# Six expert blocks of batches 0 and 1 computed inside the attention tiles of batches 2 and 3

## The chip, the core and the metric

One core of a Trainium2 chip runs the whole kernel. Its engines are TensorE (PE; its weight loads are listed as PEld), VectorE (DVE), ScalarE (ACT), GpSimd (POOL) and SyncE (SP, which here only issues DMAs). Each takes its instructions in order and waits on semaphores. The metric is the device time of one execution in microseconds (us); lower is better.

## The reference, cut to what matters

Three stages follow each other: attention, an expert layer, and a mixer. The first two:

```python
# attention: 4 batches, 8 heads, 576 tokens, head size 64
scores = scale * q @ k.T
kth = 32nd largest of each row          # only scores >= kth stay
x = softmax(scores where >= kth) @ v
# experts: per token, in order of the sequence of each batch
logits = x @ w_gate                     # 8 experts
fresh_e = argmax(logits[s])
e = fresh_e if s == 0 or sigmoid(x @ w_local) < 0.5 else prev_e
p = softmax(logits[s])
y[s] = p[e] * (relu(x[s] @ w1[e]) @ w2[e])   # 512 -> 1024 -> 512
```

The expert of a token depends on that of the token before it in its batch, and never on another batch. The mixer (a Fourier transform over tokens and channels, a normalisation and a two-layer network) reads y and is the same in both kernels.

## The kernel before, in words

**Attention** (`attention`). Batches 0 and 1 are worked on together, head by head, then batches 2 and 3. That makes 16 units (`NPAIR`) of 9 tiles of 128 query rows each, 144 tiles (`NTILE`). In each unit tiles 0 to 3 belong to the first batch, 5 to 8 to the second, and the middle one, 4, holds 64 rows of each; it comes last. For tile t: PE computes 576 scores per row (L179), ACT copies them to SBUF (L289), DVE finds the 32 largest by seven operations, four MAX8 (L356) and three MATCH_REPLACE8 (L358), POOL builds the mask (L332) and applies it (L336) to the exponentials that ACT made (L282), PE turns the result over (L199, L201), ACT copies that out (L271, L273), and PE multiplies with the values (L227). DVE works on two tiles in alternation, `top_op(c, n)` with c the pair of tiles and n from 0 to 13. After each turn PE runs four matmuls of the identity whose result nobody reads (`keep_clock`, L210). The order on each engine is the loop `body(t)` in `run`: at step t, PE does the turn of tile t, then for even t+5 the scores of the tiles t+5 and t+6 (`LQ` = 5), then the values of tile t-1. Six buffers hold scores (`NS`). Once in nine tiles PE also computes the gates (L242).

**Routing** (`routing`). When attention has ended, DVE and PE turn the logits into a table: for each block of 128 slots of one expert, which tokens it gathers and with which gate. `NBLK` is 25, the most blocks there can be.

**Experts** (`experts`). Block by block, POOL gathers 128 rows of x from DRAM, PE turns them over (L771) and computes the hidden layer (L783), ACT and DVE split hidden values and weights into two parts each, PE computes the output in three products (L796 to L798), and POOL scatters it to `y_d` and, in reverse row order, to `r_d`. The first `SURE` = 18 blocks always run; each later one runs if the routing made so many blocks.

**Weights.** SP loads those of experts 0 and 7 (8 MB, L664 and L670) at the start, and in `experts` those of the next expert when a block's expert differs from that two blocks earlier.

Of the kernel before, what the change touches and what calls it, by code (L numbers as in the profile page):

```python
# [34 lines left out]
PAD = 1 << 20  # L35
C_IM8, C_SEG, C_J, C_LATER, C_TILE = 0, E, E + E * NT, E + E * NT + NBLK, E + E * NT + NBLK + NT
C_PAD, C_ROW, C_EPS, C_POS, C_ONE, C_UP, C_ODD, CST = 240, 270, 288, 290, 418, 546, 674, 700


def attention(nc, env, q_h, k_h, v_h, vt_h):  # L40
# [4 lines left out]
    LQ, LE = 5, 2  # L45
    NS, NE, NT_ = 6, 3, 3
    ORDER = [r for p in range(MID) for r in (p, p + MID + 1)] + [MID]
# [3 lines left out]
    with ExitStack() as ctx:  # L51
# [23 lines left out]
        ps_s = [pb(f"ps_s{n}", [P, 2, 512]) for n in range(2)]  # L75
# [12 lines left out]
        s_norm = [sem(f"s_norm{b}") for b in range(2)]  # L88
        block = ctx.enter_context(nc.Block(no_gpsimd_drain=True))
        LAST = NTILE - TPP  # L90

        @block.sync
        def _(sp):
# [42 lines left out]
            for c in range(2):  # L136
                load_w1(sp, env, (0, E - 1)[c], c)
                load_w2(sp, env, (0, E - 1)[c], c)
            with sp.Fori(1, NPAIR // 2) as i:
                for b in range(2):  # L140
                    sp.wait_ge(s_qk, TPP * (2 * i + b - 1))
                    load_qk(2 * i + b, b)
                    load_mid(2 * i + b, b)
                    sp.wait_ge(s_vw, 2 * i + b - 1)
                    load_vt(2 * i + b, b)
                    sp.wait_ge(s_pv, TPP * (2 * i + b - 1))
                    load_v(2 * i + b, b)
            for m in range(NT):
                bb, r = m // TPP, m % TPP if m < TPP else ORDER[m % TPP]
                n = bb * TPP + r  # L150
                sp.wait_ge(s_norm[bb], m % TPP + 1)
                sp.dma_start(env["x_d"][n * P:(n + 1) * P, :], X[:, r, bb * DM:(bb + 1) * DM]).then_inc(env["s_xd"], 16)

        def normalise(eng, r, bb):
            x = X[:, r, bb * DM:(bb + 1) * DM].rearrange("p (h d) -> p h d", h=H)
            eng.tensor_tensor(x, x, den[:, r, H * bb:H * bb + H, None].broadcast_to([P, H, D]), ALU.mult).then_inc(s_norm[bb], 1)

        def run(body):
            for t in range(-LQ, NTILE + 2):
                body(t)  # L160
# [8 lines left out]
        def _(pe):  # L169
            def score(k, h):  # L170
                b, r = (k // TPP) % 2, ORDER[k % TPP]
                if r < MID:
                    lhsT, rows = q_sb[b][0:D, r * P:(r + 1) * P], slice(0, D)
                elif r > MID:
                    c0 = (P - HALF) + (r - MID - 1) * P
# [3 lines left out]
                return pe.matmul(ps_s[k % 2][:, h, 0:SH], lhsT, k_sb[b][rows, h * SH:(h + 1) * SH], start=True, stop=True)  # L179

            def scores(k):
                for n in (k, k + 1):
                    b, p = (n // TPP) % 2, n % TPP
                    if p == 0:
                        pe.wait_ge(s_qk_in[b], 32 * (n // (2 * TPP) + 1))
                    if ORDER[p] == MID:
                        pe.wait_ge(s_mid_in[b], 32 * (n // (2 * TPP) + 1))
                if k >= 2:
                    pe.wait_ge(s_copy, k)
                score(k, 0)  # L190
                score(k + 1, 0)
                score(k, 1).then_inc(s_qk, 1)
                score(k + 1, 1).then_inc(s_qk, 1)
# [18 lines left out]
            def values(k):  # L212
                b, r = (k // TPP) % 2, ORDER[k % TPP]
                if r == 0:
# [9 lines left out]
                lo, hi = (0, VW) if r < MID else (VW, 2 * VW) if r > MID else (0, 2 * VW)  # L224
# [20 lines left out]

            def body(t):
                if live(t):
# [14 lines left out]
        def _(act):  # L262
            act.dma_start(k_sb[0][:, :], k_h[0]).then_inc(s_qk_in[0], 16)

            def body(t):
# [19 lines left out]
                if live(k):  # L285
                    act.wait_ge(s_qk, (k | 1) + 1)
                    if k >= NS:
                        act.wait_ge(s_mask, k - NS + 1)
                    act.activation(s_sb[k % NS][:, :].rearrange("p (h c) -> p h c", h=2), ps_s[k % 2][:, :, 0:SH],  # L289
                                   ACT.Copy).then_inc(s_copy, 1)  # L290
                k = t - 1
                if live(k):
                    u, r = k // TPP, ORDER[k % TPP]
                    act.wait_ge(s_pv, k + 1)
                    for two in range(2):
                        if (two == 0 and r > MID) or (two == 1 and r < MID):
                            continue
                        rows = slice(0, P) if r != MID else slice(two * HALF, two * HALF + HALF)
                        c0 = two * VW
                        act.activation(gd[rows, r, u, :], ps_o[k % 2][rows, c0 + D:c0 + VW], ACT.Copy)  # L300
                        op = act.activation(X[rows, r, u * D:(u + 1) * D], ps_o[k % 2][rows, c0:c0 + D], ACT.Copy)  # L301
                    op.then_inc(s_o, 1)
                if gates_at(t):
# [5 lines left out]
                    act.activation(g[0:S - KC * P, KC], src[0:S - KC * P, KC], ACT.Copy).then_inc(s_vg, 1)  # L309

# [1298 lines left out]
```

## Time and profile before

| | us |
|---|---|
| median of 3 runs | 1561.29 |
| lowest and highest | 1560.42, 1561.83 |
| profiled execution | 1560.65 |
| its span, first to last instruction | 1558.8 |
| PE busy | 1417.2 (91%) |
| DVE busy | 1075.7 (69%) |
| ACT busy | 604.3 (39%) |
| POOL busy | 624.9 (40%) |
| mean granted clock of PE | 0.926 |

Busy time is an average over stages with different limits. In time, the attention's last search for maxima ends at 703.4 us, routing's first operation is at 720.0, the first block's transposes are at 743.1, the mixer's first loads are issued at 1041.0, and the span ends at 1558.8. The stage at hand has to be read by itself, from the timeline and from windows. The clock is listed as a share of 2.4 GHz: 1.00 is 2.4 GHz throughout, 0.50 is 1.2 GHz throughout.

### The profile page before, as it was taken

How to read it: one execution, taken by the hardware profiler on the slowest of the kernel's cores; microseconds unless marked ns; L12 is line 12 of the kernel's file. 1: busy time of each engine (PE TensorE's matmuls, PEld its weight loads, DVE VectorE, ACT ScalarE, POOL GpSimd, SP SyncE). 2: the span in 40 equal slices, each digit the busy share in tenths (PEclk: the TensorE clock that was granted, in tenths of full speed). 3: DMA queues.
4: the chain of work that ended last, by engine and by line, in shares of the span. 5: the costliest groups of instructions: out<-in, count | busy, mean ns of one | idle time of the engine just before them, and what ended most of it. 6: DMA issues, size and time to landing. Idle time of an engine off the chain costs nothing. (4 is left out here: it accounts for less than half of the span.)

```text
span 1558.8 us, 24264 instructions
## 1 busy us (share of the span) xinstructions
PE 1417.2 (91%) x8476; PEld 1214.2 (78%) x8476; DVE 1075.7 (69%) x2133; ACT 604.3 (39%) x1469; POOL 624.9 (40%) x502
## 2 busy tenths in 40 slices
PE   6898898989888998985999999967999999999998
PEld 4777777777677777774899999953777789999987
DVE  7999999999999999998455555546646422422222
ACT  4555455555455555541444444413322221321111
POOL 4666666666866666660244444422202100000000
PEclk9889898898999988986899999975999999999999
DMA  9110111111011011102017356442322011411111
GB/s 324 34 33 28 29 32 32 33 32 28 14 31 32 25 32 32 69 1 75 32 59 260 132 193 234 160 153 89 128 75 71 31 41 65 138 41 41 41 41 61
DMA packets 67146, 117.01 MB, mean 75 GB/s; under 512 B 27283, under 2 KB 27412, under 8 KB 67042
## 3 DMA queue, kind: packets, MB, share of 16 engines
q1 hardware_dynamic: 57306, 87.19, 16.9%
q0 software_dynamic: 8928, 27.00, 4.9%
q8 instruction: 60, 0.98, 0.3%
q10 hardware_dynamic: 808, 1.48, 0.3%
q14 instruction: 44, 0.36, 0.1%
HBM read 87.33 MB, written 30.42 MB: 76 GB/s over the span
## 5 line engine op out<-in xcount | busy, mean ns | idle before, releaser
L332 POOL TENSOR_SCALAR keep<-s_sb,top 128x576 f32<-128x576 f32 x142 | 244.4, 1721 | 224.2 <-DVE top L356 224.2
L356 DVE MAX8 top<-w_sb 128x8 f32<-128x576 f32 x432 | 304.0, 744 | 0.0
L227 PEld LDWEIGHTS ps_o<-v_sb,eT 128*128 128x128 f32 (+1 forms) x1440 | 202.0, 206 | 37.7 <-issue 26.3
L227 PE MATMUL ps_o<-v_sb,eT 128*128 128x74 f32 (+3 forms) x1440 | 225.4, 298 | 0.0
L1367 DVE SCALAR_TENSOR_TENSOR h_lo<-ps_ch,h_hi 128x384 fp32r<-128x384 f32 x96 | 53.4, 556 | 242.1 <-ACT h_hi L1218 242.0
L358 DVE MATCH_REPLACE8 w_sb<-top,w_sb 128x576 f32<-128x576 f32 x288 | 211.2, 739 | 0.0
L336 POOL TENSOR_TENSOR e_sb<-e_sb,keep 128x576 f32<-128x576 f32 x142 | 200.0, 1408 | 21.8 <-POOL keep L332 0.6
L199 PE MATMUL ps_t<-ident,e_sb 128*128 128x128 f32 x576 | 107.0, 315 | 84.4 <-POOL e_sb L336 78.7
L210 PE MATMUL ps_o<-ident 128*128 128x128 f32 x1152 | 180.5, 309 | 0.0
L210 PEld LDWEIGHTS ps_o<-ident 128*128 128x128 f32 x1152 | 167.1, 223 | 1.9 <-ACT rows L301 0.7
L783 PEld LDWEIGHTS ps_h<-bxT,w 128*128 128x128 f32 x1408 | 162.4, 194 | 3.4 <-issue 1.6
L783 PE MATMUL ps_h<-bxT,w 128*128 128x128 f32 x1408 | 162.7, 277 | 1.2 <-SPq L755 1.2
L1218 ACT ACTIVATE h_hi<-ps_ch 128x384 fp32r<-128x384 f32 x96 | 47.1, 491 | 286.6 <-PE ps_ch L1050 286.6
L199 PEld LDWEIGHTS ps_t<-ident,e_sb 128*128 128x128 f32 x576 | 68.3, 155 | 102.7 <-POOL e_sb L336 91.5
L271 ACT ACTIVATE eT<-ps_t 128x512 f32<-128x512 f32 x144 | 86.0, 597 | 140.2 <-PE ps_t L199 140.1
L1048 PE MATMUL ps_ch<-un_hi,w_hi 128*128 128x384 f32 x384 | 132.0, 344 | 1.6 <-DVE un_lo L1361 1.6
L1050 PE MATMUL ps_ch<-un_hi,w_lo 128*128 128x384 f32 x384 | 130.1, 339 | 0.0
L1049 PE MATMUL ps_ch<-un_lo,w_hi 128*128 128x384 f32 x384 | 129.6, 338 | 0.0
L824 ACT ACTIVATE w_hi<-w 128x1024 fp32r<-128x1024 f32 x88 | 85.8, 1045 | 102.8 <-PE ps_y L798 101.8
L289 ACT ACTIVATE s_sb<-ps_s 128x576 f32<-128x576 f32 x144 | 92.1, 640 | 81.5 <-PE ps_s L179 81.5
L282 ACT ACTIVATE e_sb<-s_sb,nmax 128x576 f32<-128x576 f32 x144 | 111.9, 777 | 14.3 <-ACT nmax L277 1.5
L1048 PE MATMUL ps_cy<-w_hi,h_hi 128*128 128x512 f32 x288 | 114.3, 397 | 0.0
(214 smaller groups left out, 2409.9 us busy)
## 6 DMA issues: line engine op xcount, KB each, us to landing
w<-in_w SPq DMA_DIRECT2D x18, 2048.0 KB, 13.5
stage<-in_w_ch SPq DMA_DIRECT2D x16, 512.0 KB, 3.5
q_sb<-in_q SPq DMA_DIRECT2D x16, 288.0 KB, 2.8
vT<-in_vt SPq DMA_DIRECT2D x16, 288.0 KB, 3.1
x_d<-rows SPq DMA_DIRECT2D x18, 256.0 KB, 2.4
u<-u_d SPq DMA_DIRECT2D x18, 256.0 KB, 2.9
x_d<-u POOLq DMA_DIRECT2D x18, 256.0 KB, 2.6
u<-x_d SPq DMA_DIRECT2D x18, 256.0 KB, 2.8
```

What stands on the lines that cost most here:

```text
L199: mm = pe.transpose(ps_t[:, c * P:(c + 1) * P], e_sb[k % NE][:, c * P:(c + 1) * P], ident[:, :])
L210: pe.matmul(ps_o[k % 2][:, 384:384 + P], ident[:, :], ident[:, :], start=True, stop=True)
L227: mm = pe.matmul(ps_o[k % 2][:, lo:hi], eT[k % NT_][0:n, c, :], v_sb[b][0:n, c, lo:hi], start=(c == 0), stop=(c == KC))
L282: act.activation(e_sb[k % NE][:, :], s_sb[k % NS][:, :], ACT.Exp, bias=nmax[:, k % NE:k % NE + 1], scale=SCALE).then_inc(s_exp, 1)
L332: pool.tensor_scalar(keep[t % 2][:, :], s_sb[t % NS][:, :], top[t % NS][:, TOPK - 1:TOPK], None, ALU.is_ge).then_inc(s_keep, 1)
L336: pool.tensor_tensor(e_sb[t % NE][:, :], e_sb[t % NE][:, :], keep[t % 2][:, :], ALU.mult).then_inc(s_mask, 1)
L356: dve.max(eight, src).then_inc(s_top, 1)
L358: dve.match_replace(out=w_sb[k % 2][:, :], in_to_replace=eight, in_values=src, imm_value=-BIG).then_inc(s_top, 1)
L783: mm = pe.matmul(ps_h[half][:, m, :], w1[c][:, k, f0:f0 + P], xT[c][:, k, :], start=(k == 0), stop=(k == NC - 1))
L1048: pe.matmul(out_, hi1, hi2, start=first, stop=False)
L1049: pe.matmul(out_, hi1, lo2, start=False, stop=False)
L1050: return pe.matmul(out_, lo1, hi2, start=False, stop=last)
```

## The change

Four things are new in `attention`. The routing of batches 0 and 1 (tokens 0 to 1151) is computed by a generator, `early_routing`, of which DVE takes two steps after each `top_op` from pair 38 on. PE's part of it stands at fixed places of the tiles 74 to 79 (`HOPS`). From tile 83 to 142 PE runs 105 small units, spread evenly: for each of 6 blocks (`NA`) the turn of x ("x"), 8 units of the hidden layer ("h", four matmuls of 128x128 each) and 8 of the output ("y", one matmul of 128x512), in plain float32; `keep_clock` stops at tile 83. The blocks are laid out full ones first, then partly filled ones. ACT copies the units' results and issues the loads of their weights, with the expert read from SBUF; POOL gathers and scatters.

The two banks of PSUM that the units need come from the scores: each tile has one bank now instead of two, half of a pair's scores is computed at each step, and ACT copies them in two pieces of 288 instead of one of 576. Batches 0 and 1 are normalised in the tiles 75 to 79, two a tile, and stored at once. The routing after attention treats the tokens of the second half, and gives slots of the full table to those of the first half that are in none of the six blocks. `SURE` is 12 now. The weights of experts 0 and 7 for the expert stage are loaded by ACT near the end of attention instead of by SP at the start.

```diff
+    HOPS = [(MIDDLE + n, at) for n, at in ((2, 2), (3, 2), (4, 1), (4, 2), (5, 2), (7, 2))]
...
-        ps_s = [pb(f"ps_s{n}", [P, 2, 512]) for n in range(2)]
+        ps_s = [pb(f"ps_s{n}", [P, 512]) for n in range(2)]
+        ps_a = [pb(f"ps_a{n}", [P, 512]) for n in range(2)]
...
+        UNITS = [("x", 0, 0)] + [("none", 0, 0)] * 3
+        for j in range(NA):
+            UNITS += [("h", j, m) for m in range(NF)] + [("y", j, m) for m in range(NF // 2)]
+            UNITS += [("x", j + 1, 0)] if j + 1 < NA else []
+            UNITS += [("y", j, m) for m in range(NF // 2, NF)]
+        EARLY0, EARLY1 = MIDDLE + 11, NTILE - 1
...
             def body(t):
                 if live(t):
                     if t == 0:
                         pe.wait_ge(env["s_ident"], 1)
                     turn(t)
-                    keep_clock(t)
-                if live(t + LQ) and (t + LQ) % 2 == 0:
-                    scores(t + LQ)
+                    if t < EARLY0:
+                        keep_clock(t)
+                between(t, 0)
+                k = t + LQ
+                if live(k):
+                    scores(k - k % 2, k % 2)
+                between(t, 1)
                 if live(t - 1):
                     values(t - 1)
+                between(t, 2)
...
+                if t == MIDDLE + 7:
+                    act.wait_ge(a["s_idx"], IDX_E)
+                    for j in range(2):
+                        early_w1(j)
+                        early_w2(j)
+                for unit in units_at(t):
+                    early(*unit)
...
+                if t == EARLY0 - 1:
+                    pool.wait_ge(a["s_idx"], IDX_G)
+                    pool.wait_ge(env["s_xd"], 16 * HT)
+                    for j in range(2):
+                        gather(j)
...
+            routing = early_routing()
             for c in range(NTILE // 2):
                 for n in range(14):
                     top_op(c, n)
-                if c == NTILE // 4 + 2:
-                    dve.wait_ge(s_o, NTILE // 2)
-                    invert(slice(0, TPP), 0)
+                    now[0] = (c, n)
+                    if c >= ROUTE:
+                        next(routing, None)
+                        next(routing, None)
...
-        SURE = NT
+        SURE = NT - NA
```

(`units_at(t)` gives the units of tile t, the n-th of them at place n modulo 3; `MIDDLE` is 72, `ROUTE` 38.)

The order on PE at tiles 89 and 90, before: `ps_t` is the turned tile, `ps_o` identity products and values, `ps_s` scores.

```order
L199 MATMUL ps_t<-ident,e_sb 128x128 x4
L201 MATMUL ps_t<-ident,e_sb 64x128
L210 MATMUL ps_o<-ident 128x128 x4
L179 MATMUL ps_s<-k_sb,q_sb 128x288 x4
L227 MATMUL ps_o<-v_sb,eT 128x74 x5
L199 MATMUL ps_t<-ident,e_sb 128x128 x4
L201 MATMUL ps_t<-ident,e_sb 64x128
L210 MATMUL ps_o<-ident 128x128 x4
L227 MATMUL ps_o<-v_sb,eT 128x148 x5
```

The same place now; `ps_a` takes the units' results, `stage` and `w_0` are their inputs:

```order
L363 MATMUL ps_t<-ident,e_sb 128x128 x4
L365 MATMUL ps_t<-ident,e_sb 64x128
L448 MATMUL ps_a<-stage,w_0 128x128 x4
L345 MATMUL ps_s<-k_sb,q_sb 128x288 x2
L448 MATMUL ps_a<-stage,w_0 128x128 x4
L391 MATMUL ps_o<-v_sb,eT 128x74 x5
L363 MATMUL ps_t<-ident,e_sb 128x128 x4
L365 MATMUL ps_t<-ident,e_sb 64x128
L458 MATMUL ps_a<-w_0,stage 128x512
L345 MATMUL ps_s<-k_sb,q_sb 128x288 x2
L458 MATMUL ps_a<-w_0,stage 128x512
```

The identity products are gone, four unit pieces stand in their place, and the scores are two and two instead of four at once.

The order on DVE at the start of a pair of tiles in the second half, before:

```order
L356 MAX top<-w_sb 128x8 x2
L358 MATCH_REPLACE w_sb<-top,w_sb 128x576 x2
L356 MAX top<-w_sb 128x8 x2
L358 MATCH_REPLACE w_sb<-top,w_sb 128x576 x2
L356 MAX top<-w_sb 128x8 x2
```

And now, at the start of pair 40, where the generator counts the slots of each expert:

```order
L682 MAX top<-s_sb 128x8
L733 CAST early_cnt<-ps_a 128x8
L734 TENSOR_SCALAR early_cnt<-ps_a 128x8
L682 MAX top<-s_sb 128x8
L735 TENSOR_SCALAR early_cnt<-early_cnt 128x16
L736 TENSOR_TENSOR early_cnt<-early_cnt 128x8
L684 MATCH_REPLACE w_sb<-top,s_sb 128x576
L738 SCALAR_TENSOR_TENSOR early_endb<-cst,early_cnt 128x16
L740 TENSOR_SCALAR early_full<-early_cnt 128x8
L684 MATCH_REPLACE w_sb<-top,s_sb 128x576
L741 TENSOR_TENSOR early_move<-early_endb 128x8
L742 SCALAR_TENSOR_TENSOR early_move<-early_move,early_full 128x8
```

Between one search operation and the next, two steps of the routing stand.

The order on ACT at the end of tile 79, before (`gd` and `rows` are the copies of a tile's result, `v_sb` the gates' columns):

```order
L300 ACTIVATE gd<-ps_o 128x10
L301 ACTIVATE rows<-ps_o 128x64
L308 ACTIVATE v_sb<-ps_o 128x8x9
L309 ACTIVATE v_sb<-ps_o 64x2x9
L271 ACTIVATE eT<-ps_t 128x512
L273 ACTIVATE eT<-ps_t 64x128
```

And now, where ACT reads the first blocks' experts and loads their weights:

```order
L549 ACTIVATE rows<-ps_o 128x64
L556 ACTIVATE v_sb<-ps_o 128x8x9
L557 ACTIVATE v_sb<-ps_o 64x2x9
L572 TENSOR_LOAD early_e
L572 ISA x2
L1040 ISA
L1040 DMA w_0<-in_w 128x4x1024
L580 TENSOR_LOAD early_e
L580 ISA x2
L1046 ISA
L1046 DMA w_0<-in_w 128x8x512
L572 TENSOR_LOAD early_e
```

Four such groups (two blocks, two weights each) stand between tile 79's copies and the next tile's.

## Rows read from the trace of the kernel before

**Rows 1.** Page, span in 40 slices: busy tenths, and granted clock in tenths.
```profile
PE   6898898989888998985999999967999999999998
...
PEclk9889898898999988986899999975999999999999
```

**Rows 2.** Groups by line: line, engine, op, tiles, count | busy us, mean ns | idle, releaser.
```profile
L356 DVE MAX8 top<-s_sb 128x8 f32<-128x576 f32 x144 | 100.8, 740 | 8.3 <-ACT s_sb L289 8.3
...
L783 PE MATMUL ps_h<-bxT,w 128*128 128x128 f32 x1408 | 162.7, 277 | 1.2 <-SPq L755 1.2
```

**Rows 3.** Windows of one pair of tiles: busy by engine, PEclk, DMA share.
```profile
481.10:490.80 9.70, 7.18 (x56) 6.14 (x56) 9.70 (x21) 5.04 (x15) 6.24 (x4) 1.00 0.00 0
...
548.60:558.20 9.60, 7.49 (x38) 6.92 (x38) 9.60 (x21) 3.32 (x10) 6.23 (x4) 0.64 0.01 2
...
sum 298.80, PE 263.48 PEld 223.40 DVE 298.80 ACT 156.64 POOL 199.35; mean PE 8.50 PEld 7.21 DVE 9.64 ACT 5.05 POOL 6.43
```

**Rows 4.** Timeline, two tiles at the full clock: start, length, engine, line, op, tiles.
```profile
567.55 0.66 PE L199 MATMUL ps_t<-ident,e_sb 128*128 128x128 f32 x4
...
568.15 1.06 PE L210 MATMUL ps_o<-ident 128*128 128x128 f32 x8
...
568.42 1.39 DVE L356 MAX8 top<-s_sb 128x8 f32<-128x576 f32 x2
...
569.14 1.24 PE L179 MATMUL ps_s<-k_sb,q_sb 64*128 64x288 f32 x8
...
570.31 1.49 PE L227 MATMUL ps_o<-v_sb,eT 128*128 128x74 f32 x10
...
571.72 0.66 PE L199 MATMUL ps_t<-ident,e_sb 128*128 128x128 f32 x4
...
573.22 1.38 PE L227 MATMUL ps_o<-v_sb,eT 128*128 128x74 f32 x10
...
574.53 0.66 PE L199 MATMUL ps_t<-ident,e_sb 128*128 128x128 f32 x4
...
578.06 1.39 DVE L356 MAX8 top<-s_sb 128x8 f32<-128x576 f32 x2
```

**Rows 5.** Timeline of PE: gates; scores of a pair with the middle tile.
```profile
578.71 1.29 PE L242 MATMUL ps_o<-wg_sb,vT 128*128 128x18 f32 x10
...
682.15 0.75 PE L179 MATMUL ps_s<-k_sb,q_sb 64*128 64x288 f32 x2
...
684.78 1.38 PE L227 MATMUL ps_o<-v_sb,eT 128*128 128x74 f32 x10
```

**Rows 6.** Timeline of PE in the experts: the next block's transposes, twice.
```profile
1002.23 0.60 PE L771 MATMUL ps_bx<-ident,x 128*128 128x128 f32 x4
...
1015.27 0.60 PE L771 MATMUL ps_bx<-ident,x 128*128 128x128 f32 x4
```

**Rows 7.** Timeline of DVE: logits, and small operations of routing.
```profile
705.49 0.83 DVE L369 TENSOR_TENSOR part<-gd,den 128x648 f32<-128x648 f32 x1
...
706.35 1.31 DVE L371 TENSOR_REDUCE lg<-part 128x81 f32<-128x648 f32 x1
...
726.74 0.17 DVE L604 TENSOR_SCALAR cnt_i<-cnt_i 128x8 int32<-128x8 int32 x1
...
726.95 0.18 DVE L605 TENSOR_TENSOR_SCAN endb<-cst,cnt_i 128x8 f32<-128x8 f32 x1
...
727.44 0.30 DVE L608 SCALAR_TENSOR_TENSOR place<-endb,ps_r 128x144 f32<-128x144 f32 x1
```

**Rows 8.** Timeline of SP's queue: weight loads issued back to back.
```profile
14.73 0.51 SPq L670 DMA_DIRECT2D w<-in_w  x1
...
15.28 5.65 SPq L664 DMA_DIRECT2D w<-in_w  x1
...
20.98 2.44 SPq L670 DMA_DIRECT2D w<-in_w  x1
```

**Rows 9.** Timeline of PE, last tiles of attention.
```profile
696.58 1.12 PE L199 MATMUL ps_t<-ident,e_sb 128*128 128x128 f32 x4 [3.50 <-POOL e_sb L336]
```

More of the change, by code:

```diff
@@ L88, in attention, with units_at, unit_tile @@
         s_norm = [sem(f"s_norm{b}") for b in range(2)]
+        s_rt = sem("s_rt")
+        r, a = choice_buffers(nc, ctx, "_a", ps_a), early_buffers(nc, ctx, env)
+        a["s_yo"] = env["s_early"]
         block = ctx.enter_context(nc.Block(no_gpsimd_drain=True))
         LAST = NTILE - TPP
+        cst = env["cst"]
+        ones, below = cst[:, C_ONE:C_ONE + P], cst[:, C_UP:C_UP + P]
+        NF = F // P
+        UNITS = [("x", 0, 0)] + [("none", 0, 0)] * 3
[4 more added lines that the diff above has]
+        EARLY0, EARLY1 = MIDDLE + 11, NTILE - 1
+        def units_at(t):
+            at = lambda x: min(max(len(UNITS) * (x - EARLY0) // (EARLY1 - EARLY0), 0), len(UNITS))
+            return UNITS[at(t):at(t + 1)]
+        def unit_tile(unit):
+            return next(t for t in range(EARLY0, EARLY1) if unit in units_at(t))
         @block.sync
@@ new lines, in early_inverse, with early_x @@
+            def early_inverse():
+                pe.wait_ge(r["s_go"], WHAT)
+                for n in range(HT):
+                    pe.wait_ge(r["s_go"], POS + n + 1)
+                    mm = pe.matmul(ps_a[1][:, 0:2 * NA], a["at_pos"][:, n, :], a["what"][:, n, :, :].rearrange("p a j -> p (a j)"),
+                                   start=(n == 0), stop=(n == HT - 1))
+                mm.then_inc(r["s_back"], 1)
+            def early_x(j, bank):
+                pe.wait_ge(a["s_x"][j % 2], 16 * (j // 2) + 16)
+                if j > 0:
+                    pe.wait_ge(a["s_h"], 2 * j)
+                else:
+                    pe.wait_ge(a["s_idx"], IDX_GATE)
+                for k in range(KC):
+                    mm = pe.transpose(bank[:, k * P:(k + 1) * P], env["x"][j % 2][:, k * P:(k + 1) * P], ident[:, :])
+                mm.then_inc(a["s_t"], 1)
@@ new lines, in between @@
+            def between(t, at):
+                if (t, at) == HOPS[0]:
+                    choice_turn(pe, r, ident)
+                elif (t, at) == HOPS[1]:
+                    choice_ends(pe, r, ident)
+                elif (t, at) == HOPS[2]:
+                    choice_row(pe, r, ones)
+                elif (t, at) == HOPS[3]:
+                    choice_last(pe, r, ident)
+                elif (t, at) == HOPS[4]:
+                    early_rank()
+                elif (t, at) == HOPS[5]:
+                    early_inverse()
+                for n, unit in enumerate(units_at(t)):
+                    if n % 3 == at:
+                        early(*unit)
@@ L404, in _ @@
                     op.then_inc(env["s_lg"], 1)
-            for r in ORDER[early:]:
-                normalise(dve, r, 1)
+            for rt in ORDER[early:]:
+                normalise(dve, rt, 1)
 def wait_apart(eng, s, value, idle):
```

559 lines of the change are left out of this document (408 added, 151 removed).

## The prediction

> **What bounds the kernel now.** I read the slices first. In the attention, the first 18 of 40 slices, PE's digits are 8 and 9 and its clock's too [rows 1], so both PE and DVE look full. The groups by line settle which of them sets the pace. The searches for maxima never wait except once, 8.3 us at the start [rows 2]; windows of 9.6 us show DVE busy for all of each and PE for 8.50 of 9.64 on the mean [rows 3]. One pair of tiles takes DVE 578.06 - 568.42 = 9.64 us [rows 4], and 72 pairs make 694 us. DVE bounds the attention, and work that is put on it there costs its full length.
>
> In the experts it is PE: two blocks' transposes stand 1015.27 - 1002.23 = 13.04 us apart [rows 6], with no gap of PE between. The hidden layer's group has 1408 instructions [rows 2] at 64 a block (two for each float32 matmul, 32 matmuls), so 22 blocks run. The mixer comes after all of this and is not touched.
>
> **Blocks that go.** The tables are decided by the inputs. By the reference on the drawn inputs the tokens of the eight experts are 418, 244, 288, 356, 217, 167, 276, 338, which makes 22 blocks, as the trace has. Of batches 0 and 1 they are 242, 119, 157, 178, 78, 77, 147, 154. The six blocks are the full ones of experts 0, 2, 3, 6 and 7 and the partly filled one of expert 0, with 114. What is left is 176, 244, 160, 228, 217, 167, 148, 210: two blocks each, 16. Six blocks go, 6 x 13.04 = -78.2 us. More expert changes stall only if loads come late; the loads come every fourth block, while a load of two weights has the time of about a block and a half, as before. The nine conditional blocks that are skipped at the end, three before, cost some branches beside a POOL that is still scattering: 0 to 1 us, I take 0.3.
>
> **DVE in the attention.** The generator adds 69 operations (the inversion of the sums was in the loop before). Two are the logits, from after the loop: 0.86 us from the one's start to the other's [rows 7], and 1.31. The other 67 are small. In routing such an operation takes 0.17 to 0.18, and 0.21 from start to start in a dependent row [rows 7]; those with 128x144 outputs take 0.30, and here they are 128x72. I count 30 narrow ones at 0.18, 28 at 0.24 (half-width tables, reductions, scans) and the 9 comparisons with 128 positions at 0.22: 14.1 us. With the logits +16.3. From below, an operation lies partly under the next: two searches of 0.74 [rows 2] take 1.39 together [rows 4], so 0.05 to 0.09 of each could hide: 12. From above, each waits for the one before it, +0.06 each: 21. PE's answers that DVE waits for are due one to several searches later than PE can reach its place by my count from pair 37 on, so I charge nothing for them; 3 if one is late. The logits' old place at the end lay beside PE's last tiles and gives nothing back.
>
> **PE in the attention, tiles 83 to 142.** This is the term on which all hangs. At the full clock, a pair takes PE 574.53 - 567.55 = 6.98 us, of which the identity products are 569.14 - 568.15 = 0.99 a tile [rows 4]. That leaves 5.00. Gates add 1.29 in nine tiles [rows 5], 0.29 a pair. A middle tile among the scores makes them 684.78 - 682.15 = 2.63 [rows 5] instead of 570.31 - 569.14 = 1.17 [rows 4], 0.32 a pair. A "h" unit is 8 instructions of the hidden layer, 8 x 162.7/1408 = 0.92 us [rows 2]; a "y" unit has as many columns and fewer weight loads, so 0.92 at most; turning x is 0.6 [rows 6]. A block is 16 x 0.92 + 0.6 = 15.3 us, six are 92, over 30 pairs 3.06. Two groups of scores a pair instead of one cost one more change of row groups, 0.2. Sum: 5.00 + 0.29 + 0.32 + 3.06 + 0.2 = 8.9 us, against 9.64 of DVE. It fits by 0.7 us a pair, at the full clock.
>
> How much delay does DVE bear? The second half of a pair's scores is computed now at the even tile, after POOL's mask of that tile. From the timeline I place the copy about 6 us after the start of the pair before, so about 3.5 us ahead of need. A lag of PE under 3.5 us is free, and what is longer stalls DVE.
>
> The clock decides whether it fits. Before, single pairs show 1.00, and one shows 0.64 [rows 3]; the page's digits are 8 and 9 [rows 1]. The drop near the end comes after PE waited 3.50 us for POOL [rows 9]. With PE busy for more of each pair, waits of that kind get shorter. I take the clock at about 0.97, at which 8.9 becomes 9.2, and charge 5 us for pairs in which gates, middle tile and a low stretch meet. From below 0. From above, a pair at 0.82 would take 10.9, 1.2 us over DVE's, 36 us over 30 pairs.
> The Trainium skill ("TensorE: Matmul & The Clock Gate", on what actually happens) has the clock fall after idling and return with sustained work. The row of the 3.50 us wait agrees, and by that rule this term would be 0.
>
> **ACT and the weight loads.** ACT issues four loads of 2 MB in a row at tile 79. On SP's queue such issues took 0.51 us, then 5.65 and 2.44 [rows 8]: an issue can hold its engine. ACT executes in order, so eT of tile 80, the exponential of tile 82 and the scores of pair 42 queue behind it; PE waits for the first, POOL for the second, DVE for the third. ACT is free for them between 2 and 11 us after the expert numbers come, which are due early in pair 41; pair 42 starts some 11 us later. I take a stall of 3, of 0 to 6. Later loads come one at a time and take 0.5.
> The Trainium skill ("DMA: Bandwidth & Descriptors", on issuing engines that are no separate queues) calls the time to initiate a DMA usually small beside the DMA. The row of 5.65 us speaks against it; by the rule this term would be 0.
>
> The scores' copy is two of 288 columns instead of one of 576, one more instruction a tile on an engine that is busy for 5.05 of 9.64 us [rows 3]: nothing. POOL has 9.64 - 6.43 = 3.2 idle us a pair [rows 3], which holds two normalisations or a gather.
>
> **Ends.** At the start PE's second half waits for ACT's copies of the first: +0.7 (0 to 1.5), a copy and a short matmul group. At the end, tiles 140 to 142 carry six "y" units, 5.5 us, where four tiles had 4 x 0.99; the clock is low there after the wait of 3.50 us [rows 9], which doubles part of it, and ACT issues the last load before it copies tile 143: +3 (0 to 6). Routing afterwards works on half-width tables but with the same number of steps: 0 (-2 to +1).
>
> **The sum.** -78.2 + 0.3 + 16.3 + 5 + 3 + 0.7 + 3 = -49.9. The profiled execution took 1560.65, so 1510.8; the median before is 1561.29, 0.6 higher. I forecast 1511.
>
> **Rivals.**
> (a) PE becomes the bound in the tiles 83 to 142. For it: only 0.7 us of 9.64 is spare, and the mean over windows before is 8.50 busy with less work [rows 3]. Against it: those 8.50 include low clock and identity products. If the clock stays at about 0.86 there, a pair takes 10.3, +20 us: about 1531. Chance 0.17.
> (b) Slower than before. The same mechanism with the low clock for most of the stretch: without the identity products, PE waits at each even mask, falls to half speed, and works at it for the rest of the pair. It decides against the change from the point where a pair costs 50/30 = 1.7 us more than forecast, 11.3 us, a mean clock of 0.79. At 0.72 a pair is 12.4 and the kernel 1589. For it: a pair at 0.64 exists [rows 3]. Against: in the next highest idle case, 7.18 busy, the clock was 1.00. Chance 0.03.
> (c) The stage of experts does not shrink as said: a block more is left (rounding in the logits moves a token over an edge), or ifs and weight loads stall PE. Of what is left, expert 1 with 244 is nearest to a third block, 13 tokens away. One block is +13: 1524. Chance 0.03.
> (d) It is cheaper than I say: the added operations hide better and PE never lags: -78.2 + 12 + 3 = 1497. Chance 0.15.
> The forecast itself, 1503 to 1520, has 0.62.
>
> **Numbers.** The range that holds 8 in 10 takes in most of the cheap case (d) and of (a), whose upper bound of 36 us would end at 1542: 1494 to 1540. A measurement of this kernel can tell 0.2%, 3 us, from no change. Only (b) ends above 1558, and a part of it between: faster 0.95, same 0.01, slower 0.04.
>
> **What would show it.** In the profile after: 16 blocks, 1024 instructions of the hidden layer, 13.0 us apart. The last search ends near 703 + 25 = 728. Small operations between the searches sum to 16 us in the pairs 38 to 42. In the second half of the tiles, windows show DVE busy for all or nearly all of each pair; if its searches wait for ACT's scores by more than 10 us in sum, (a) holds, and the granted clock of the stretch tells whether by clock or by work. A gap of ACT right behind the four loads shows their price. What would make it wrong most easily is PE's sum of 8.9: a few tenths more in each pair take all the spare time.

## The result and the profile after

| | before | after |
|---|---|---|
| median, us | 1560.86 (1559.59 to 1561.83) | 1522.06 (1512.85 to 1523.24) |
| ratio of the times | 1 | 0.9741, 95% interval 0.9707 to 0.9775 |
| profiled execution, its span | 1560.65, 1558.8 | 1512.85, 1511.0 |
| mean granted clock of PE, profiled | 0.926 | 0.933 |

The change takes 38.8 us off the median; the forecast was 1511, in a range of 1494 to 1540. So the time lies in the range, but the gain is 11 us short of the forecast's 49.9. The profiled execution, 1512.85, is the fastest of the four, and the other three took 1521.2 to 1523.2 at a mean clock of 0.923 to 0.926 (two more on record, not in the median, took 1517.3 and 1524.4). So there are two questions: what the trace is made of, and what it does not contain.

The page of the changed kernel, PE's busy tenths and its granted clock in 40 slices, answers [rows 1]:

```profile
PE   6889889989879999999679999847999999999998
...
PEclk9989998998779999999779999956999999999999
```

The two sevens in a row early on are the 11th and 12th slice, 378 to 453 us. There the early routing runs, between the searches of the tiles 76 to 83. From there to the end of the attention the clock is 9 or more.

The groups by line, the ones that answer to [rows 2] and the two new ones of the units:

```profile
L682 DVE MAX8 top<-s_sb 128x8 f32<-128x576 f32 x144 | 103.2, 769 | 10.7 <-ACT s_sb L538 10.6
...
L1159 PE MATMUL ps_h<-bxT,w 128*128 128x128 f32 x1024 | 119.5, 278 | 1.2 <-SPq L1131 1.2
...
L448 PE MATMUL ps_a<-stage,w 128*128 128x128 f32 x384 | 53.6, 283 | 0.0
L458 PE MATMUL ps_a<-w,stage 128*128 128x512 f32 x96 | 51.0, 618 | 0.0
```

The hidden layer has 1024 instructions, 16 blocks. The searches waited 10.6 us for score copies, 8.5 of them at the start; only 2.07 are new. A search reads 769 ns in place of 740, yet a pair of tiles takes what it took. Windows of one pair of tiles each in the second half answer to [rows 3]:

```profile
477.33:486.97 9.64, 9.64 (x61) 6.79 (x59) 9.64 (x22) 6.16 (x20) 6.24 (x5) 1.00 0.41 141
544.79:554.43 9.64, 8.30 (x52) 5.77 (x50) 9.64 (x22) 5.16 (x17) 6.25 (x5) 1.00 0.08 29
...
670.10:679.74 9.64, 9.64 (x50) 6.19 (x50) 9.64 (x22) 4.91 (x17) 6.25 (x5) 1.00 0.51 198
```

DVE is busy for the whole of each pair, the clock is 1.00, and a pair is 9.64 us as before. PE reads as full in two of them and is still not the bound: the searches never wait here, and a run below puts PE's own work at 8.9 us a pair.

Where the new waits are, in a list of DVE's waits from 370 to 750 us (what waits, for whom, us in total, times, longest):

```profile
DVE early_cnt L733 <- PE ps_a L415: 2.2, 1, 2.2
DVE spread_a L127 <- PE ps_a L81: 2.1, 1, 2.1
DVE top L682 <- ACT s_sb L538: 2.1, 1, 2.1
...
DVE early_oh L133 <- PE ps_a L87: 0.4, 1, 0.4
```

Three are the early routing's waits for PE, 4.75 us, and the fourth stands behind ACT's four weight loads. Their timeline:

```profile
427.04 0.24 ACT L556 ACTIVATE v_sb<-ps_o 128x72 f32<-128x72 f32 x1 [10.25 <-PE ps_o L406]
...
428.41 0.43 ACTq L1040 DMA_DIRECT2D w<-in_w  x1
429.56 0.40 ACTq L1046 DMA_DIRECT2D w<-in_w  x1
430.65 3.17 ACTq L1040 DMA_DIRECT2D w<-in_w  x1
434.51 2.09 ACTq L1046 DMA_DIRECT2D w<-in_w  x1
436.71 0.60 ACT L518 ACTIVATE eT<-ps_t 128x512 f32<-128x512 f32 x1 [9.38 <-issue]
```

The experts' blocks are 13.04 us apart, as in [rows 6]:

```profile
776.43 0.60 PE L1147 MATMUL ps_bx<-ident,x 128*128 128x128 f32 x4
...
789.47 0.60 PE L1147 MATMUL ps_bx<-ident,x 128*128 128x128 f32 x4
```

And the stage's end, the last scatter of POOL and the first loads of the mixer, first the changed kernel, then the kernel before:

```profile
981.19 0.97 POOL L1257 DMA_INDIRECT r_d<-y,at_y  x1 [0.30 <-issue]
992.36 1.99 SPq L1346 DMA_DIRECT2D xa<-y_d  x3
```

```profile
1037.58 0.98 POOL L881 DMA_INDIRECT r_d<-y,at_y  x1 [0.30 <-issue]
1041.00 1.30 SPq L970 DMA_DIRECT2D xa<-y_d  x3
```

From 982.16 to 992.36 are 10.2 us, where before there were 2.4. PE's last matmul had ended at 977.7, and no engine has a row in those 10.2 us. This is called the gap below.

The traces side by side, by milestones:

| stretch | before | after | difference | forecast |
|---|---|---|---|---|
| to the first search | 7.86 | 8.56 | +0.7 | +0.7 |
| first search to the last one's end | 695.6 | 719.5 | +23.9: 17.1 operations, 4.75 waits for PE, 2.07 behind ACT | +16.3, 0, +3, and +5 for PE |
| last search to routing's first operation | 16.5 | 13.7 | -2.8 | +3 |
| routing, to the first block | 23.1 | 22.7 | -0.4 | 0 |
| experts, to the end of POOL's last scatter | 295.5 | 217.7 | -77.8 | -78.2 |
| gap before the mixer | 2.4 | 10.2 | +7.8 | +0.3 |
| mixer | 517.8 | 518.7 | +0.8 | 0 |
| span | 1558.8 | 1511.0 | -47.8 | -49.9 |

### The profile page after: what moved, and what is told of

It reads as the page before. It is cut to its first block and busy times, and to the rows that moved or that the text cites. A ratio compares the mean times of both kernels' runs of the same rounds, so it can differ in the third digit from the quotient of the medians.

```text
span 1511.0 us, 23165 instructions
## 1 busy us (share of the span) xinstructions
PE 1376.4 (91%) x7974; PEld 1127.9 (75%) x7974; DVE 1049.7 (69%) x2158; ACT 596.6 (39%) x1596; POOL 613.8 (41%) x493
## 3 DMA queue, kind: packets, MB, share of 16 engines
q8 instruction: 65, 1.06, 0.3%
## 5 line engine op out<-in xcount | busy, mean ns | idle before, releaser
L682 DVE MAX8 top<-w_sb 128x8 f32<-128x576 f32 x432 | 311.3, 774 | 0.1
L391 PEld LDWEIGHTS ps_o<-v_sb,eT 128*128 128x128 f32 (+1 forms) x1440 | 191.7, 195 | 59.9 <-issue 47.2
L391 PE MATMUL ps_o<-v_sb,eT 128*128 128x74 f32 (+3 forms) x1440 | 217.4, 290 | 0.0
L363 PE MATMUL ps_t<-ident,e_sb 128*128 128x128 f32 x576 | 100.9, 301 | 63.9 <-POOL e_sb L659 52.3
L345 PE MATMUL ps_s<-k_sb,q_sb 64*128 64x288 f32 x512 | 119.5, 496 | 7.0 <-DMA k_sb<-in_k 4.6
L1159 PEld LDWEIGHTS ps_h<-bxT,w 128*128 128x128 f32 x1024 | 119.2, 195 | 2.9 <-issue 1.6
L1159 PE MATMUL ps_h<-bxT,w 128*128 128x128 f32 x1024 | 119.5, 278 | 1.2 <-SPq L1131 1.2
L538 ACT ACTIVATE s_sb<-ps_s 128x288 f32<-128x288 f32 x288 | 104.8, 406 | 38.8 <-PE ps_s L345 38.3
L1426 PE MATMUL ps_cy<-w_hi,h_lo 128*128 128x512 f32 x288 | 113.3, 394 | 0.0
L1425 PE MATMUL ps_cy<-w_lo,h_hi 128*128 128x512 f32 x288 | 113.1, 393 | 0.0
## 6 DMA issues: line engine op xcount, KB each, us to landing
w<-in_w SPq DMA_DIRECT2D x12, 2048.0 KB, 10.9
```

The costliest lines, as they stand in the source:

```text
L345: return pe.matmul(ps_s[k % 2][:, 0:SH], lhsT, k_sb[b][rows, h * SH:(h + 1) * SH], start=True, stop=True)
L363: mm = pe.transpose(ps_t[:, c * P:(c + 1) * P], e_sb[k % NE][:, c * P:(c + 1) * P], ident[:, :])
L391: mm = pe.matmul(ps_o[k % 2][:, lo:hi], eT[k % NT_][0:n, c, :], v_sb[b][0:n, c, lo:hi], start=(c == 0), stop=(c == KC))
L682: dve.max(eight, src).then_inc(s_top, 1)
L1159: mm = pe.matmul(ps_h[half][:, m, :], w1[c][:, k, f0:f0 + P], xT[c][:, k, :], start=(k == 0), stop=(k == NC - 1))
L1425: pe.matmul(out_, hi1, lo2, start=False, stop=False)
```

## Experiments

Each time is a median, and the kernel before, measured beside each, had medians of 1560.2 to 1560.5. The changed kernel itself came first.

**The changed kernel again.**

> The changed kernel once more, for a second trace. Its other executions stood 4 to 12 us above the profiled one (1512.85) with a lower mean granted clock (0.921 to 0.927 against 0.933). Theory A: in the slower ones the clock falls in more windows of tiles 83 to 142, PE's pair then passes 9.64 us and the searches wait: DVE's waits after 450 us rise from none to 5 to 10 us, and the last search ends at 733 to 738 instead of 728.0. Theory B: the attention is the same (728 within 1 us) and the difference lies in the mixer or the expert stage, the block distance staying 13.04. The gap from the end of POOL's last scatter (982.16) to the mixer's first loads (992.36) is 10.2 again by both.

Measured: 1519.71 (1509.53 to 1526.04), ratio 0.9754 (0.9730 to 0.9778). Its trace was again of the fastest execution, so it could decide nothing on the other runs. The gap was 9.3 us, not 10.2. Its waits for PE in the early routing were 1.2 us where the first trace had 4.75: that term moves from execution to execution.

**The skipped blocks.** Two kernels with nested conditional blocks, on all engines and on PE alone:

```diff
-            for j in range(SURE, NBLK):
-                with eng.If(used > j):
-                    body(j // 2, j % 2)
+            def rest(j):
+                with eng.If(used > j):
+                    body(j // 2, j % 2)
+                    if j + 1 < NBLK:
+                        rest(j + 1)
+
+            rest(SURE)
```

> Each conditional block from the 13th on stands inside the one before it, on all engines, so that one jump ends the stage where nine were taken. Theory A (the skipped blocks cost the 7.8 us that the gap before the mixer has grown by): the gap of 10.2 us falls to 2.4 or less, and the time falls by 7 to 8 us against the changed kernel in the same call. Theory B (the gap is the landing of the scatters or the stage's barrier): it stays at 10 us and the time is the same within 2 us.

> The same nesting on PE alone; DVE, ACT, POOL and SP still jump over nine blocks one by one. PE's last matmul ends at 977.7 and the mixer starts 14.7 us later, which is 1.6 us a skipped block if PE is the last; before it was 7.0 us for three, with POOL's scatter ending 2.4 us before the mixer. Theory A (PE's jumps set the end): the gap falls to 2.4 to 4 us, as with all engines nested. Theory B (POOL's own jumps behind its scatter set it, 0.9 us each): it stays at 10 us. If it falls by 1 to 5 us, two engines are near each other.

Measured: all engines 1504.08, ratio 0.9650 (0.9633 to 0.9667); PE alone 1507.16, 0.9679 (0.9649 to 0.9710). POOL's last scatter and the mixer's first loads, nested on all engines, then on PE alone:

```profile
979.78 0.97 POOL L1261 DMA_INDIRECT r_d<-y,at_y  x1 [0.30 <-issue]
983.30 1.42 SPq L1350 DMA_DIRECT2D xa<-y_d  x3
```

```profile
980.24 0.97 POOL L1266 DMA_INDIRECT r_d<-y,at_y  x1 [0.30 <-issue]
984.97 1.31 SPq L1355 DMA_DIRECT2D xa<-y_d  x3
```

The gap is 2.55 and 3.76 us. So PE's jumps made most of it, and those of the other engines are worth 1.2 us more. The control, nested on POOL alone:

> The nesting on POOL alone; PE jumps over nine blocks one by one, as in the changed kernel. Theory A (PE's jumps set the gap, and the repeated runs spread with them): the gap is 9 to 10.5 us, the median 1517 to 1521 and the highest run above 1522, as in the changed kernel and unlike the two kernels whose PE is nested (medians 1504.1 and 1507.2). Theory B (any change of the program's code removes the spread, or it was luck): the median is 1510 to 1513.

Measured: 1515.13 (1511.95 to 1517.59), ratio 0.9713 (0.9700 to 0.9727). The gap was 10.9 us (981.93 to 992.85): it stays, as theory A has it, 0.4 us over the range given. The median lies between the ranges of both theories, and no run was above 1518, so PE's jumps alone do not bring the spread of the repeated runs. The same question put to the kernel before:

```diff
+            for _ in range(more):
+                with eng.If(used > NBLK - 1):
+                    body((NBLK - 1) // 2, (NBLK - 1) % 2)
...
-            blocks(pe, used, body)
+            blocks(pe, used, body, more=6)
```

> The kernel before, with six more conditional blocks on PE alone, never taken, behind its own three. Theory A (PE jumps over a conditional block at 1.3 to 1.6 us each, and the kernel before hides three of them beside POOL's scatter): the gap from the end of POOL's last scatter to the mixer's first loads goes from 2.4 us to 10 us, and the time is 7 to 8 us above the kernel before. If the repeated runs spread by 10 us and more here as well, where those of the kernel before lie within 3.9 us (1558.67 to 1562.56), the spread too comes of the jumps. Theory B (the jumps were dear in the changed kernel only for its place in memory or its early blocks): the time is that of the kernel before within 2 us.

Measured: 1570.11 (1569.03 to 1570.65), ratio 1.0064 (1.0050 to 1.0078), which is 9.8 us more, and a spread of 1.6 us. In its trace:

```profile
1036.76 0.99 POOL L884 DMA_INDIRECT r_d<-y,at_y  x1 [0.30 <-issue]
1049.95 2.14 SPq L973 DMA_DIRECT2D xa<-y_d  x3
```

A gap of 12.2 us. PE's last matmul had ended at 1033.2; nine jumps and the stage's end took 16.8 us, and with three they took 7.0 at most (1034.0 to 1041.0, set by POOL's scatter). Six jumps are thus worth at least (16.8 - 7.0) / 6 = 1.6 us each. The jumps do not take the same time in every execution. With nine of them the time from PE's last matmul to the mixer's first loads is 12.8 to 16.5 us in the traces of the changed kernel and its variants (14.7 in the first one), and 7.0 with one, again set by POOL. In the first trace that makes between (14.7 - 7.0) / 8 = 1.0 and 14.7 / 9 = 1.6 us for each.

**The waits for PE in the early routing.** First by the clock, then by the order.

```diff
-                for _ in range(4):
+                for _ in range(12 if MIDDLE + 1 <= k < EARLY0 else 4):
```

> Twelve clock-keeping matmuls in place of four in each of tiles 73 to 82, nothing else. In the changed kernel DVE waited 2.12, 0.40 and 2.23 us for PE there (399.11, 402.61, 408.77) and PE itself 3.71 us for DVE, at a granted clock of 0.55 to 0.68. Theory A (the waits come of the low clock, that came of PE's idling while the searches of a pair take 13 to 16 us): the clock stays at 1.0 from 380 to 440 us, the waits fall from 4.75 us to under 1.5, and the last search ends 3 to 4 us earlier (724 to 725). Theory B (the waits are of the order of the instructions: each hop stands behind a turn and a values step): the waits stay at 4 to 5 us or rise by the 1 to 2 us that the added matmuls take.

Measured: 1521.83 (1516.64 to 1527.84), ratio 0.9764 (0.9729 to 0.9799). The waits did not fall: those for PE were 5.1 us (3.6 and 1.5), and those behind ACT rose to 5.8 over that stretch. But the clock was not held either. The windows of 380 to 390 and 410 to 420 us showed 1.00, 390 to 400 still 0.69, so this run does not part the two theories cleanly. The last search ended at 734.9; 2.7 us of that come from one pair of the first half, which took 12.35 us while PE was at 0.50 (it comes up again below). Then the places of the waits:

```diff
-    HOPS = [(MIDDLE + n, at) for n, at in ((2, 2), (3, 2), (4, 1), (4, 2), (5, 2), (7, 2))]
-    AWAIT = [(ROUTE + n, at) for n, at in ((0, 9), (1, 0), (1, 7), (1, 10), (2, 0), (3, 4))]
+    HOPS = [(MIDDLE + n, at) for n, at in ((2, 2), (3, 2), (4, 1), (4, 2), (5, 2), (8, 1))]
+    AWAIT = [(ROUTE + n, at) for n, at in ((0, 9), (1, 0), (1, 10), (1, 13), (2, 3), (3, 9))]
```

> The four later waits of DVE for PE's answers in the early routing stand three to five searches later, and PE's inversion two places later (tile 80 in place of 79); the rest is the changed kernel, whose two traces show 4.75 and 1.2 us of such waits (spread_a, early_oh, early_cnt) and its last search ending at 728.06 and 726.93. Theory A (the waits are of the order: the answer comes one to three searches after it is asked for, more when the clock is low; more clock-keeping matmuls made it worse): the three waits fall to under 0.5 us in sum, the last search ends at 725 to 726.5 with the wait behind ACT's loads (1.9 to 2.1 us) left, and the repeated runs, 1509.5 to 1526.0 for the changed kernel, lie closer, with a median 5 us or more lower. Theory B (the waits are not what makes the runs differ): the sum falls all the same but the median stays within 2 us of the changed kernel's 1519.7 to 1522.

Measured: 1518.18 (1514.81 to 1524.22), ratio 0.9741 (0.9720 to 0.9763). The three waits are gone, and one has grown, in DVE's waits of this kernel from 370 to 750 us:

```profile
DVE top L682 <- ACT s_sb L538: 5.0, 1, 5.0
```

The gain was given back: the five pairs from the 38th on took 73.32 us, and 73.33 in the changed kernel. The searches come to this place 2.8 us earlier, but the expert numbers that ACT waits for in tile 79 do not (426.9 us, 427.3 in the changed kernel), and ACT is through with its loads at 436.8 (436.7). That takes 2.9 us back; the other 1.8 went into operations that took longer. The last search ended at 729.0, not at the 725 to 726.5 of theory A, and by the median theory B holds. So both were taken together, with the nesting:

```diff
-                if t == MIDDLE + 7:
-                    act.wait_ge(a["s_idx"], IDX_E)
-                    for j in range(2):
-                        early_w1(j)
-                        early_w2(j)
+                if t == MIDDLE + 8:
+                    act.wait_ge(a["s_idx"], IDX_E)
+                    early_w1(0)
+                if t == MIDDLE + 9:
+                    early_w2(0)
+                if t == MIDDLE + 10:
+                    early_w1(1)
+                if t == MIDDLE + 11:
+                    early_w2(1)
```

> Together: the nested conditional blocks on all engines (1503.34 to 1508.72 by themselves), the later waits of the run hops, and ACT's four weight loads at tiles 80, 81, 82 and 83, one each, in place of all at tile 79. Theory A (each takes away its own wait): the wait of the searches for ACT's score copy (1.9 to 2.3 us in four traces) goes, the last search ends at 723.5 to 724.5, the gap before the mixer is 2.5 us, and the time is 1499 to 1501, 3 us below the nested kernel. Theory B (a load that comes later makes PE wait for the first expert's weights or for the gathered rows at tiles 83 to 85, and DVE with it): DVE has a new wait of 2 us or more between 430 and 460 us, and the time is that of the nested kernel, 1503 to 1506.

> The combined kernel again, for a trace without the long low-clock stretch: its first trace (1511.34) had PE at a clock of 0.50 from 254 to 288 us, a tile of PE at 6.78 us where the searches of a tile take 4.82, and three pairs of 12.49, 13.56 and 12.12 us; its other runs were 1499.24 to 1506.87. Theory A (that stretch alone set that run apart): a trace without it has all pairs up to 370 us at 9.64 us, the last search ends at 725 to 727, and the time is 1499 to 1502; a second trace with it lies 8 to 10 us above. Theory B: runs differ in the expert stage or the mixer, and a fast run has its last search at 735 as well.

Measured: 1502.38 (1499.24 to 1511.34), ratio 0.9619 (0.9603 to 0.9636), and 1501.08 (1499.57 to 1509.00), ratio 0.9635 (0.9615 to 0.9654). It is the fastest version here. The second trace is of 1499.57: DVE has no wait between 370 and 720 us, the five pairs take 69.18 us, the last search ends at 723.8, a little earlier than forecast, and the gap is 2.5 us.

The first trace is of the run at 1511.34, the only one of the longer runs that was seen from inside. Its last search ended at 735.2. Windows of half a pair from 249.64 us, and the five turns of PE in that stretch:

```profile
249.64:254.46 4.82, 3.11 (x19) 2.85 (x18) 4.82 (x11) 1.48 (x6) 4.52 (x4) 0.72 0.00 0
254.46:259.28 4.82, 4.82 (x18) 3.55 (x16) 4.82 (x11) 1.66 (x4) 1.71 (x2) 0.50 0.01 3
...
268.92:273.74 4.82, 4.82 (x20) 3.65 (x19) 2.05 (x5) 1.60 (x5) 4.38 (x3) 0.50 0.01 3
...
283.38:288.20 4.82, 4.82 (x20) 3.61 (x19) 2.83 (x7) 1.09 (x5) 3.10 (x2) 0.50 0.00 0
...
293.02:297.84 4.82, 4.82 (x38) 3.93 (x35) 2.45 (x6) 3.31 (x10) 3.26 (x3) 1.00 0.01 3
```

```profile
252.53 1.11 PE L363 MATMUL ps_t<-ident,e_sb 128*128 128x128 f32 x4 [1.71 <-POOL e_sb L663]
...
260.26 1.12 PE L363 MATMUL ps_t<-ident,e_sb 128*128 128x128 f32 x4
...
267.04 1.12 PE L363 MATMUL ps_t<-ident,e_sb 128*128 128x128 f32 x4
...
273.82 1.12 PE L363 MATMUL ps_t<-ident,e_sb 128*128 128x128 f32 x4
...
280.60 1.12 PE L363 MATMUL ps_t<-ident,e_sb 128*128 128x128 f32 x4
```

After a wait of 1.71 us for POOL, PE works at 0.50 (1.2 GHz) for 34 us of whole windows without a pause, about 41 us with the parts of the windows at both ends. A tile takes it 6.78 us, a pair 13.56, and the pairs of the searches take 12.49, 13.56 and 12.12 us there, 9.25 over three of 9.64. In the trace of the kernel nested on all engines the clock fell in the same place (0.50 from 254.46) and was at 0.94 from 264.10 on; no search waited. The shorter form is in the run with more clock-keeping: 0.50 in the windows from 138.32 to 152.78 us and 0.78 in the next, and its pair of 12.35 us.

**PE's spare time, and the clock-keeping.**

```diff
-                    if t < EARLY0:
-                        keep_clock(t)
+                    keep_clock(t)
```

> The changed kernel with the four clock-keeping matmuls a tile kept in tiles 83 to 143 too, beside the expert units. PE is busy 8.6 to 8.9 us of a pair's 9.64 there, and eight matmuls of a pair take 2.1 us at full clock (1.06 a tile). Theory A (PE has a spare of 0.7 to 1.0 us a pair and no more): a pair becomes 10.7 to 11.0 us, the 30 pairs take 32 to 41 us more, the last search ends at 760 to 768 us, and the time is 1545 to 1560. Theory B (part of PE's busy time is the lengthened reading of matmuls that stand in a queue, and the spare is larger): the last search ends below 745 us.

Measured: 1551.56 (1550.41 to 1555.43), ratio 0.9949 (0.9933 to 0.9965). The pairs from the 46th to the 69th took 261.41 us, 10.89 each at a clock of 1.00, and the last search ended at 759.3, 0.7 us short of the range. PE is busy in all windows of that stretch and the searches wait 31 us for score copies, so PE sets the pace there. Less the identity products, 0.99 in each of its two tiles, PE's pair is 8.9 us, the forecast's number. The opposite, no identity products in the first half of the combined kernel:

```diff
-                for _ in range(4):
+                for _ in range(4 if k >= MIDDLE else 0):
```

> The combined kernel without clock-keeping matmuls in tiles 0 to 71. At the low clock a tile of PE is 6.78 us, 1.92 of them clock-keeping, so without them 4.86 to 4.94, near the 4.82 of the searches; at the high clock 1.06 us a tile less. Theory A (the clock-keeping makes a low-clock stretch longer than the searches, and the searches wait): no pair up to 370 us takes over 11 us however long the clock is low, and the repeated runs lie within 4 us, at 1499 to 1503. Theory B (PE idles more, the clock is low through the first half, and the tiles with gates, 2.2 us more at the low clock, make the searches wait each time): the first half takes 10 us or more longer, the last search ends above 735, and the time is 1508 to 1525.

Measured: 1513.16 (1506.26 to 1514.51), ratio 0.9688 (0.9671 to 0.9705), at a mean clock of 0.881 in the profiled run: 12 us over the combined kernel. Theory B holds. Two windows of a pair there:

```profile
324.60:334.20 9.60, 9.60 (x39) 7.54 (x40) 8.94 (x19) 3.76 (x15) 6.19 (x5) 0.50 0.01 2
...
343.80:353.40 9.60, 9.60 (x30) 6.48 (x29) 7.88 (x17) 4.94 (x14) 5.19 (x4) 0.50 0.00 0
```

**The end of the attention.**

```diff
-                for _ in range(4):
+                for _ in range(10 if k >= NTILE - 7 else 4):
```

> The kernel before, with ten clock-keeping matmuls in place of four in each of its last seven tiles. There PE ran at a granted clock of 0.50 from 694.5 to 703.4 us and the stretch from the last search to the routing's first operation was 16.6 us (703.4 to 719.96); in the changed kernel it was 13.8 us at a clock of 1.00 with the expert units in place of the clock-keeping. Theory A (the clock alone made the tail shorter, by 2.8 us): here too the clock is 1.00 around the last search, the stretch is 13.5 to 14.5 us, the last search still ends within 1 us of 703.4, and the time is 2 to 3 us under the kernel before. Theory B (it is the order of the last operations, normalising before the logits of late tiles): the stretch stays at 16 us or grows with the 2 us of added matmuls.

Measured: 1561.38 (1559.30 to 1563.26), ratio 1.0007 (0.9996 to 1.0017): no change. The clock was 1.00 from 684 to 716 us, yet the stretch was 16.0 us (702.90 to 718.92). Theory A fell. What sets this stretch is DVE: it waits for no matmul in it, in this run, in the kernel before and in the changed one, so PE's added products (2.40 us in each tile where the four took 1.06) cost nothing. The kernel before, then the changed kernel:

```profile
704.75 0.82 DVE L384 SCALAR_TENSOR_TENSOR e_sb<-s_sb,top,e_sb 128x576 f32<-128x576 f32 x1 [0.58 <-ACT e_sb L282]
...
707.70 0.18 DVE L363 TENSOR_SCALAR den<-gd 128x24 f32<-128x24 f32 x1
```

```profile
727.92 1.81 DVE L817 SCALAR_TENSOR_TENSOR e_sb<-s_sb,top,e_sb 128x576 f32<-128x576 f32 x2
729.65 0.17 DVE L689 TENSOR_SCALAR den<-gd 128x24 f32<-128x24 f32 x1
```

In the kernel before, the two logit operations of [rows 7], 0.83 and 1.31 us, stand between these two rows. In the changed kernel they are gone from this place, since it computes them earlier. DVE is busy for 12.2 us of the stretch where it was for 14.3, which is 2.1 of the 2.8 us. The rest is mostly the wait of 0.58 us for ACT, which the added products removed here too. PE can still come to set this stretch: with units and identity products both, in the run above that kept them to the end, it was 18.7 us, 5.0 of them waits for ACT.

## Why the prediction came out as it did

- **Six blocks, -78.2: right.** 16 blocks, 13.04 us apart, -77.8.
- **The skipped blocks, +0.3 in bounds of 0 to 1: the mis-sized term,** +7.8 in the trace. "Some branches beside a POOL that is still scattering" took the jumps to be all but free, and looked at the wrong engine. PE needs 1.0 to 1.6 us for each in the first trace. Nine of them outlast POOL's 4.5 us of scattering, and three do not. Shown in both directions: against the first trace's 10.2 us, nested blocks take 7.6 us of the gap away, PE's alone 6.4, and six more in the kernel before cost 9.8.
- **DVE's operations, +16.3 in bounds of 12 to 21: right,** 17.1 in the first trace (17.5 in its five pairs alone). In the combined kernel's second trace, which has no waits there, the five pairs took 69.18 where the kernel before needs 49.05, so there it is 20.1. What differs is how small operations meet a tensor operation of POOL (below): in that trace two comparisons are held up by 1.2 us each, in the first trace one operation is.
- **Hops, "I charge nothing; 3 if one is late": wrong,** 4.75 and 1.2 in two traces. Three waits stood too close behind their questions. Moving them removed the waits, but their time came back until ACT's loads were spread too.
- **PE's lag, +5 in bounds of 0 to 36: the mechanism was right and its place was not.** The sum of 8.9 us a pair held (10.89 less 1.98 in the run with identity products kept), and no search from tile 86 on waited in the changed kernel's trace. So the 5 us were not paid there. A price of this kind came in the first half instead, with the identity products still in: in the one slow trace of the combined kernel the long stretch at 0.50 makes PE slower than the searches, +9.3. The forecast looked for low clock only where the units are.
- **ACT's loads, +3 in bounds of 0 to 6: right,** 2.07 (and 5.0 where the numbers come later). The four issues and their reads held ACT for 9.4 us.
- **The tail, +3: wrong in sign,** -2.8. The step that failed is "the logits' old place at the end lay beside PE's last tiles and gives nothing back": DVE sets that stretch, and without the logits it is 2.1 us less busy in it. The low clock of [rows 9], which was to make PE's units dear, did not count, since DVE does not wait for PE there.
- **Start, routing: right** within 0.4.

In the trace the errors cancel: +7.5 for the jumps, +4.75 for the hops and +0.8 each for DVE's operations and the mixer, against -5.8 for the tail, -5 for PE and -0.9 for ACT; 0.4 each for routing and the blocks cancel, and 2.1 are left. That the trace came within 2 us of the forecast, and its last search at 728.0 as said, is therefore luck. The other 9 us of the median are runs with a lower mean clock, and no trace shows such a run of this kernel.

What stays open is why the changed kernel's runs have long stretches at the low clock more often. The kernel before stayed within 4 us (1558.67 to 1562.56) in all its runs; of 39 runs of the kernels with the change (those with altered clock-keeping from tile 83 on or in the first half not counted), 13 lay 7 to 17 us above the fastest of their kernel. The long stretch was seen inside one run only. Shorter ones are in every trace: in the first half, stretches at 0.50 of 10 us or more number 3 or 4 in each of the ten traces with the change and with the identity products there, and 2, 1 and 0 in the three traces of the kernel before and its variants. Those of 10 to 14 us cost the searches 0 to 0.9 us, one of 17 us cost 2.7 (0.6 in the kernel before), and one of 41 us cost 9.3. So with the change long stretches are more frequent already before its early blocks begin, and the one of 17 us cost more. The split of the scores is the part of it that is present there, and it was not undone by itself; that it is the cause is not shown. The two nested kernels' medians lie 15.6 and 12.6 us below the changed kernel's of the same series, but the gap explains only 6.7 and 5.5 (9.3 us in the changed kernel's trace of that series). Their fastest runs lie 6.2 and 4.6 below its fastest, about as much as the gap; for the rest of the medians no cause was shown.

## What to carry to other kernels

A conditional body that is skipped is not free: on PE it took 1 to 1.6 us and more here, and a row of them should be nested, so that one jump ends it. Place a wait for another engine's answer as far behind the question as the slow case needs, and then look at what else comes next, since the gain of a removed wait can go at once to the next one (with the 4.75 us of hops gone, the wait behind ACT's loads grew from 2.07 to 5.0 us). When work is moved away from the end of a stage, ask which engine sets that end: if it is the one that did the work, the move gives something back (2.1 us here). And forecast the low clock where the engine idles now and where its work at half speed is longer than the pace of the others, over the whole stage, not only where the work is added.

## What the runs showed of the hardware

- A jump of PE over a conditional body of 60 matmuls of the program took 1.6 us or more in the kernel before with six more of them, and between 1.0 and 1.6 us in the changed kernel's first trace.
- A masking operation of POOL holds up small operations of DVE. In the combined kernel's second trace, DVE's comparisons and POOL's masks:

```profile
418.27 1.60 DVE L773 TENSOR_SCALAR early_at_pos<-cst,early_pos 128x128 f32<-128x128 f32 x2
418.37 1.43 POOL L663 TENSOR_TENSOR e_sb<-e_sb,keep 128x576 f32<-128x576 f32 x1
...
420.47 0.46 DVE L773 TENSOR_SCALAR early_at_pos<-cst,early_pos 128x128 f32<-128x128 f32 x2
...
421.58 1.61 DVE L773 TENSOR_SCALAR early_at_pos<-cst,early_pos 128x128 f32<-128x128 f32 x2
421.64 1.48 POOL L663 TENSOR_TENSOR e_sb<-e_sb,keep 128x576 f32<-128x576 f32 x1
```

  Two comparisons take 0.46 us by themselves and 1.60 when POOL's masking has begun beside them: the second ends 0.07 us after POOL's operation. In the changed kernel an operation on 1x96 took 1.46 in this way, ending 0.11 us after POOL's. The searches for maxima beside such maskings kept their 0.74 and 0.75 us. The Trainium skill ("SBUF — State Buffer", on who interferes with whom) has DVE's second pair of ports shared with GpSimd: a DVE operation with two inputs in SBUF contends for it, and copies, casts and tensor_scalar operations can, in their 2-port modes, where whoever issues first holds the pair for the whole instruction. These rows agree in that the comparisons end with the masking; in which mode they ran no trace shows.
- Identity products that do no work bought 12 us in the first half. Without them the clock was 0.50 over whole pairs and the mean of the run 0.881; with them the mean was 0.938.
